# GpSimd's step of the first layer in another order, extra operands in even steps, and the last mish half by half

## The reference, cut to what matters

```python
x = attention(q, k, v)                # 4 x 8 heads, 576 x 64, block causal: x is 2304 x 512
h = x @ w_in                          # layer 0, w_in 512 x 2048
x = (h * clip(h + 3, 0, 6) / 6) @ w_out      # w_out 2048 x 512
h = x @ w2_in                         # layer 1
out = (h * tanh(log1p(exp(h)))) @ w2_out     # mish
```

## Time and profile before

| | |
|---|---|
| median of 3 runs | 976.23 us (974.47 to 979.89) |
| the profiled execution's own time | 974.51 us |
| its span, first to last instruction | 972.7 us |
| TensorE busy | 950.8 us, 98% |
| VectorE, ACT, GpSimd busy | 720.8, 667.9, 412.5 us |
| granted clock of TensorE | 0.998 |
| DMA | 216.43 MB, 223 GB/s in the mean |

### The profile page before, as it was taken

The page is one execution under the profiler, slowest core; times in us unless marked ns, Lnnn a source line. Parts: engine busy times, 40 slices in busy tenths (PEclk is TensorE's granted clock), DMA queues, the critical chain, the costliest instruction groups (busy, mean ns, idle before and its releaser), DMA issues.

```text
span 972.7 us, 17753 instructions
## 1 busy us (share of the span) xinstructions
PE 950.8 (98%) x6028; PEld 848.1 (87%) x6028; DVE 720.8 (74%) x1393; ACT 667.9 (69%) x1479; POOL 412.5 (42%) x386
## 2 busy tenths in 40 slices
PE   7999999999999999999999999999999999999998
PEld 7898888999887888889889989888988998988896
DVE  7898898786859667676757677777877777777654
ACT  7999999754445565565646567777776877776653
POOL 7899879666837577676936360000000000000000
PEclk9999999999999999999999999999999999999999
DMA  7988888658798988888765646555655654564255
GB/s 215 269 242 250 255 262 241 173 148 246 245 303 281 289 280 281 240 284 262 253 227 200 226 149 217 184 195 195 223 195 178 240 203 153 184 249 184 90 193 195
DMA packets 84602, 216.43 MB, mean 223 GB/s; under 512 B 10144, under 2 KB 16928, under 8 KB 84512
## 3 DMA queue, kind: packets, MB, share of 16 engines
q1 hardware_dynamic: 84368, 215.01, 67.4%
q10 hardware_dynamic: 144, 0.29, 0.1%
HBM read 162.07 MB, written 39.92 MB: 208 GB/s over the span
## 4 chain that ended last, share of the span: by engine, by line
PE 86%; DVE 6%; ACT 2%; POOL 2%; DMA 2%; issue 1%; SPq 0%; ACTq 0%; DVEq 0%
PE psum L1033 36%; PE psum L916 11%; PE psum L918 11%; PE psum L917 11%; PE psum L861 5%; PE psum L840 5%; PE psum L820 4%; PE psum L821 3%; DMA ext_d<-ext_made 2%; POOL xlo L1899 1%; DVE xlo L1575 1%; DVE ebuf L1640 1%; POOL osplit L1912 1%; DVE glo L1646 1%; ACT ghi L1305 0%
## 5 line engine op out<-in xcount | busy, mean ns | idle before, releaser
L1033 PE MATMUL psum<-ghi,osplit 128*128 128x512 f32 (+1 forms) x640 | 216.4, 372 | 1.3 <-POOL osplit L1912 1.3
L916 PE MATMUL psum<-xhi,whi 128*128 128x256 f32 (+1 forms) x640 | 187.8, 293 | 7.9 <-POOL xlo L1899 4.5
L918 PE MATMUL psum<-xhi,wlo 128*128 128x256 f32 (+1 forms) x640 | 187.1, 292 | 0.0
L917 PE MATMUL psum<-xlo,whi 128*128 128x256 f32 (+1 forms) x640 | 186.9, 292 | 0.0
L1033 PE MATMUL psum<-osplit,ghi 128*128 128x512 f32 x576 | 180.9, 395 | 1.1 <-DVE glo L1646 0.8
L1912 POOL TENSOR_TENSOR osplit<-oraw,osplit 128x512 fp32r<-128x512 f32 x80 | 119.1, 1492 | 119.4 <-ACT osplit L1224 119.2
L1646 DVE SCALAR_TENSOR_TENSOR glo<-ebuf,ghi 128x512 fp32r<-128x512 f32 x144 | 125.4, 871 | 30.8 <-ACT ghi L1305 22.8
L916 PEld LDWEIGHTS psum<-xhi,whi 128*128 128x128 f32 x640 | 121.3, 190 | 20.6 <-POOL xlo L1899 5.0
L1033 PEld LDWEIGHTS psum<-ghi,osplit 128*128 128x128 f32 x640 | 118.0, 189 | 17.5 <-issue 1.7
L917 PEld LDWEIGHTS psum<-xlo,whi 128*128 128x128 f32 x640 | 121.2, 189 | 10.8
L1305 ACT ACTIVATE ghi<-ebuf 128x512 fp32r<-128x512 f32 x144 | 90.0, 625 | 50.1 <-DVE ebuf L1640 31.3
(11 more groups left out here) (123 smaller groups left out, 2118.0 us busy)
## 6 DMA issues: line engine op xcount, KB each, us to landing
ext<-ext_d SPq DMA_DIRECT2D x56, 768.0 KB, 4.4
osplit<-o_d SPq DMA_DIRECT2D x80, 512.0 KB, 5.3
oraw<-in_w_out SPq DMA_DIRECT2D x80, 256.0 KB, 5.4
wraw<-in_w_in SPq DMA_DIRECT2D x26, 512.0 KB, 5.9
ext_d<-ext_made SPq DMA_DIRECT2D x32, 384.0 KB, 6.2
attn_t<-ostage SPq DMA_DIRECT2D x32, 288.0 KB, 3.9
qkin<-in_qk SPq DMA_DIRECT2D x30, 288.0 KB, 3.7
kparts<-kparts SPq DMA_DIRECT2D x30, 288.0 KB, 4.1
```

The source lines that it names most:

```text
L916: pe.matmul(dst, hi, xh, start=(start and cc == 0), stop=False, skip_group_check=True)
L917: pe.matmul(dst, hi, xl, start=False, stop=False, skip_group_check=True)
L918: last = pe.matmul(dst, lo, xh, start=False, stop=(stop and cc == 1), skip_group_check=True)
L1033: last = pe.matmul(bank(Y_BANK + c, n), stat, mov, start=(first and m == 0), stop=(final and m == 2), skip_group_check=True)
```

## The change

GpSimd's step in the first layer (layer 0 in the code) gets another order. Before: first W_out split, products of the extra operands, first half of the x work (sums or parts or remainders), second split, second half of the x work, other splits. After, from step 1 on: x parts, the first two remainders, first split, products, the other remainders, all other splits, and last the sums with their scalings. Step 0 keeps its order. The products and with them the whole w_in job go from odd steps 11 to 25 to even steps 12 to 26, the look-ahead pieces 8 to 15 from even steps 12 to 26 to odd steps 11 to 25, and the two kinds exchange their `wraw` buffers; the waits on these buffers follow. In the second last step VectorE finishes the first half of the last mish before it goes on with the second.

```diff
-EXTRA0_STEP, EXTRA1_STEP, RES1_STEP = 3, 11, LAYER - 9
-AHEAD_STEP = [2 + t if t < 8 else EXTRA1_STEP + 1 + 2 * (t - 8) for t in range(FT)]
+EXTRA0_STEP, EXTRA1_STEP, RES1_STEP = 3, 12, LAYER - 9
+AHEAD_STEP = [2 + t if t < 8 else EXTRA1_STEP - 1 + 2 * (t - 8) for t in range(FT)]
+def next_blocks(s):
+    steps = [(blk, s - (FIRST_STEP[blk] - 2)) for blk in range(2, LATE_X)]
+    return [(blk, t, 0) if t < -4 else (blk, t - 4, 1) for blk, t in steps]
 def w_slot(m):
-    return 0 if 2 * PAIRS <= m < 3 * PAIRS else m % 2
+    return 1 if 2 * PAIRS <= m < 3 * PAIRS else m % 2
 def ahead_raw(t):
-            return hbuf[t % 2][:, 0:D] if t < 8 else wraw[1][:, t % 2 * D:(t % 2 + 1) * D]
+            return hbuf[t % 2][:, 0:D] if t < 8 else wraw[0][:, t % 2 * D:(t % 2 + 1) * D]
 # SyncE, load_w(m)
-                if m == 3 * PAIRS + 1:
+                if m == 3 * PAIRS:
                     sp.wait_ge(ahead_lo, FT)
 # SyncE, load_ahead(t)
                 elif t in (8, 9):
-                    sp.wait_ge(w_lo, own(2 * PAIRS))
+                    sp.wait_ge(w_lo, own(2 * PAIRS - 1))
 # VectorE, mish_period(s)
-                if now:
+                if s + 2 == STEPS:
+                    times_r(s + 1, 0)
+                    better_r(s + 1, 0)
+                    mish_times_h(s + 1, 0)
+                    times_r(s + 1, 1)
+                    split_g_lo(s + 1, 0)
+                    better_r(s + 1, 1)
+                elif now:
                     times_r(s + 1, 0)
                     better_r(s + 1, 0)
                     times_r(s + 1, 1)
                 if quads:
                     add_c12(s + 2)
-                if now:
+                if s + 2 < STEPS:
                     mish_times_h(s + 1, 0)
                     better_r(s + 1, 1)
                     split_g_lo(s + 1, 0)
 # GpSimd; scale_next_x, mix_next_x, next_x_lo are next_x, taken apart by kind
             for s in range(STEPS):
                 todo = [i for i in splits_at(s) if i < SPLIT_OS]
+                if s == 0:
+                    ...
+                    continue
+                mix_next_x(s)
+                next_x_lo(s, 0)
                 for i in todo[:1]:
                     split_o(i)
-                if s == 0:
-                    add_x(1, 3)
-                    scale_x(1, 3)
                 for m in jobs_at(s):
                     if JOBS[m][0] == 1 and JOBS[m][3]:
                         mix_late(m)
-                next_x(s, 0)
-                for i in todo[1:2]:
-                    split_o(i)
-                if s == 0:
-                    mix_x(1, 1)
-                next_x(s, 1)
-                for i in todo[2:]:
+                next_x_lo(s, 1)
+                for i in todo[1:]:
                     split_o(i)
+                scale_next_x(s)
```

More of the change, by code:

```diff
@@ L1913, in split_o, with scale_next_x, mix_next_x, next_x_lo @@
                                         ).then_inc(o_lo, 1)
[L1915 to L1922, removed]
-                    if t == -7 and blk < NBL:
-                        add_x(blk, part + 2 * cc)
-                        scale_x(blk, part + 2 * cc)
-                    if t == -6 and part == 0:
+            def scale_next_x(s):
+                for blk, t, cc in next_blocks(s):
+                    if t == -7 and blk < NBL:
+                        for k in range(2):
+                            add_x(blk, k + 2 * cc)
+                            scale_x(blk, k + 2 * cc)
+            def mix_next_x(s):
+                for blk, t, cc in next_blocks(s):
+                    if t == -6:
                         mix_x(blk, cc)
[L1928 to L1931, removed]
+            def next_x_lo(s, part):
+                for blk, t, cc in next_blocks(s):
+                    if t == -5:
                         for i in range(2 * part, 2 * part + 2):
@@ L1949, in _ @@
                 todo = [i for i in splits_at(s) if i < SPLIT_OS]
+                if s == 0:
+                    split_o(todo[0])
+                    add_x(1, 3)
+                    scale_x(1, 3)
+                    split_o(todo[1])
+                    mix_x(1, 1)
+                    for i in todo[2:]:
+                        split_o(i)
+                    continue
+                mix_next_x(s)
+                next_x_lo(s, 0)
                 for i in todo[:1]:
                     split_o(i)
-                if s == 0:
-                    add_x(1, 3)
-                    scale_x(1, 3)
                 for m in jobs_at(s):
```

## The result

| | before | after |
|---|---|---|
| median of 4 runs | 975.35 us (973.35 to 979.89) | 964.38 us (961.66 to 965.96) |
| ratio, with its 95% interval | | 0.9874 (0.9841 to 0.9906) |
| the profiled execution's own time | 974.51 us | 965.96 us |
| its span | 972.7 us | 964.0 us |

The ratio means 12.3 us off, 9.2 to 15.5. Forecast were 6.8 us off, 969.4, with a range from 965.5.

The account below looks back on a forecast made before the run. TensorE bounds the kernel, busy 950.8 of 972.7 us. Terms 5.2 + 0.8 + 1.6 + 0.6 - 1.4 = 6.8 us off 974.51 gave 967.7, as a median 969.4; range 965.5 to 975.5.

Parts of the forecast that it names:

- Block entries: First matmuls of blocks 3, 4, 5: TensorE's waits for GpSimd's x remainders go, 2.33 + 2.2 + 0.65 = 5.2 us gained.
- The price in odd steps: Steps 13, 17, 21, 25: ext remainder meets GpSimd's x remainders and delays M3, 0.35 us each, 1.4 us lost.
- the full price: Upper end in those four odd steps: VectorE disturbed as in step 16, up to 1.3 us each, 5.2 in all.
- M3 in even steps: Steps 12, 16, 20: M3's waits for ACT's copy, 1.1 us together, shrink as ext remainders move away; 0.8 us gained.
- Block 2: Entry of block 2: TensorE's 2.43 us wait for VectorE shrinks through earlier ext stores; 1.6 us gained, bounds 0 and 2.43.
- the named chain: Steps 3 to 10: earlier W_out splits make the ext store about 3 us sooner, a lead passed on to step 10.
- The end: Last mish: its first half comes 0.60 us sooner, cutting TensorE's 0.78 us wait for the low half of g; 0.6 gained.
- The cover of the moved loads and splits: Around step 17: later W_out splits keep 4 us of cover, the load of tile 46 keeps 3 us; no cost.
- Rival 2: Everything that is late goes, with no price in odd steps: 9.3 us off, 966.9; chance 0.18.

Follow-up runs that it names:

- end_only: The kernel before with only the last step's mish done half by half as in the kernel after: 976.22 us, ratio 0.9980.
- new_to_10: The kernel before with GpSimd's new order in steps 1 to 10 only: 975.74 us, ratio 0.9974.
- order_only: The kernel after with the ext jobs back in odd steps and the old end, so GpSimd's new order alone: 965.49 us, ratio 0.9868.
- after_again: The changed kernel, unaltered, measured once more beside other kernels: 963.27 us, ratio 0.9865.

## Why the prediction was wrong

**Block entries (5.2 us): the mechanism was right, the size wrong.** All four stops went and the remainders came when they should (397.04; said were 397.1 to 398.5; GpSimd's sum from x on was 23.1 us, said: 23.3), the products ended at 388.0 (said: 388.6), x no longer held GpSimd up. The term that was mis-sized is the price of a stop. I set it to its idle time. In the profile of before that was 4.5 us for blocks 3 and 4 together, but their sections took 12.9 + 10.6 + 12.9 + 12.1 = 48.5 us against 41.9 in after, 6.6 us; in the other two profiles with these stops 10.1 and 8.9. In runs, the clock alone gives **2.6 to 3.0 us** (3.1 - 0.5 and 3.6 - 0.6) that stand nowhere in my sum. I also took one profile's stops for typical; those of end_only were 3.17 and 2.24, of new_to_10 2.32 and 3.04.

**The price in odd steps (1.4 us): none is paid.** In step 17 of the kernel after, ACT (last x high parts, conversion, high half of g, copy for M3) and VectorE (look-ahead piece of step 16, ext remainder and relu6 of step 17):

```profile
387.48 1.15 ACT L1225 ACTIVATE xhi<-xst 128x512 fp32r<-128x512 f32 x2
...
388.52 0.84 ACT L1184 ACTIVATE ext_made<-wraw 128x768 fp32r<-128x768 f32 x1
...
391.53 0.63 ACT L1312 ACTIVATE ghi<-ebuf 128x512 fp32r<-128x512 f32 x1 [0.89 <-DVE ebuf L1647]
...
392.07 0.37 ACT L1251 ACTIVATE hbuf<-psum 128x256 f32<-128x256 f32 x1
```

```profile
378.49 1.78 DVE L1577 TENSOR_TENSOR staged<-wraw,staged 128x512 fp32r<-128x512 f32 x1
...
389.39 0.96 DVE L1552 TENSOR_TENSOR ext_made<-wraw,ext_made 128x768 fp32r<-128x768 f32 x1 [1.08 <-ACT ext_made L1184]
...
390.26 1.23 DVE L1647 SCALAR_TENSOR_TENSOR ebuf<-ebuf,hbuf 128x512 f32<-128x512 f32 x1
```

TensorE's M3 of that step:

```profile
393.12 0.28 PE L923 MATMUL psum<-xhi,ext 128*128 128x256 f32 x1
```

VectorE starts the remainder at 389.39 rather than at 390.0, as ACT is 0.7 us earlier: step 16 has lost its own delay. This wins no room, since TensorE is earlier by as much (M3 at 393.12, said: 393.8). What wins it is the short disturbance: the remainder takes 0.96 and relu6 1.23, while the small remainders are on GpSimd, less than the 2.05 and 1.78 of the earlier trace rows. I had said so, and had 1.1 us of room; the copy comes at 392.07 and ends 0.7 us ahead of M3, which doesn't wait. To take a third of the full price was an average between two cases; the rows spoke for the lower end.

**M3 in even steps (0.8):** gone, all three, 1.1 us; rather more, since order_only shows 1.31 at step 12.

**Block 2 (1.6):** gone. Its size was a matter of the execution, 0.95 us on average, not 2.43. The order of steps 1 to 10 is worth 2.5 us by the times (both ways), of which step 10, where the named chain ends, holds about 1.2.

**The end (0.6):** not seen. The wait for the low half was 0.31 in after and 0.85 in after_again, 0.86 in order_only with the old end. From step 70 to the last matmul it is 12.5 us before, 12.6 and 12.7 after; on the mean of all profiles 12.55 with the old end (4) and 12.34 with the new one (10, from 12.0 to 12.8), so it is worth 0.2 us if anything.

**The cover of the moved loads and splits:** loads, split tiles 42 and 43, the load of tile 46: no wait of TensorE came from them, as said.

**The sum once more**, in runs: 5.8 for the entries (mean stops of three profiles, 2.6 + 2.5 + 0.65), 2.6 to 3.0 clock, 1.2 to 2.5 for steps 1 to 10, 1.1 M3, 0 in odd steps and at the end: 10.7 to 12.4, measured 12.3. Rival 2, all that is late goes, was what happened, and it too left out the clock. The two parts aren't additive: order alone has 0.9868, even steps alone 0.9888, both 0.9865 to 0.9874, since the order alone leaves no idle time at a block entry, and the even steps alone at most 0.6 us (and the 1.25 at M3 of step 17), and the clock in the 10 us windows around blocks 3 and 4 is 1.00 in both.

## What to carry to other kernels

A stop of an engine with a granted clock has two prices, its idle time and the stretch at half clock that can follow it; ask for the clock in windows of a few microseconds around each stop, because a page's mean over a 24 us slice hides it. A stop that has become shorter may only have moved: at block 3 the even steps alone took it from 2.3 us to 0.6, but 1.25 us came up ahead of it in the same step, and the two sections together won 0.3 us. So compare whole sections. And a stop measured in one execution is a sample; the spread between runs of the same kernel (972.49 to 982.03 us, against 961.66 to 965.96 without the stops) is itself a sign of such stops.

## What the runs showed of the hardware that I had not expected

- The same kernel's runs differ by its stops: 972.49 to 982.03 us over 23 runs of before, with mean clocks of 1.000 and 0.992; 961.66 to 965.96 over the eight runs of the kernel after, with 0.998 to 1.000. With eight stops of 0.97 us the mean clock stayed at 1.000 in 12 runs; of eight stops of 2.63 to 2.81 us six were followed by a fall; of eight of 4.0 to 4.2 us all were.
- A 128x512 memset on GpSimd takes 0.5 us (three in 1.57), an addition 1.3; sixteen memsets a step beside full work of the other engines cost nothing (963.30).
- Attention, the same code in all kernels, took between 198.2 and 202.3 us, so a difference of two spans of single executions is uncertain by 4 us here before any change.
